# Expert rows fetched as quarters and turned by VectorE, inner rows turned among the products, attention products by form

## What is computed

```
attention:  state = gamma[h] * state + k_t v_t^T;   y_t = q_t state / sqrt(64)
experts:    e = argmax(x @ w_gate)
            out = softmax(x @ w_gate)[e] * sigmoid(x @ w_output_gate)[e] * (relu(x @ w1[e]) @ w2[e])
            w1: 8 x 512 x 1024, w2: 8 x 1024 x 512
last layer: xn = x / rms(x) * rms_g;   out = (silu(xn @ w_gate) * (xn @ w_val)) @ w_out, width 1536
```

## Time and profile before

| | us |
|---|---|
| median of 3 runs | 1125.27 |
| the runs | 1123.5 to 1125.32 |
| the profiled execution, its own time | 1125.38 |
| its span, first to last instruction | 1123.6 |
| TensorE busy in it | 1105.0 (98%) |
| attention, to the first expert product | 0 to 152 |
| expert tiles | 152 to 521 |
| last layer | 522 to the end |

### The profile page before, as it was taken

The page is one execution under the profiler, slowest core; times in us unless marked ns, Lnnn a source line. Parts: engine busy times, 40 slices in busy tenths (PEclk is TensorE's granted clock), DMA queues, the critical chain, the costliest instruction groups (busy, mean ns, idle before and its releaser), DMA issues.

```text
span 1123.6 us, 20317 instructions
## 1 busy us (share of the span) xinstructions
PE 1105.0 (98%) x6371; PEld 915.7 (81%) x6372; DVE 428.5 (38%) x804; ACT 378.3 (34%) x613; POOL 178.3 (16%) x245
## 2 busy tenths in 40 slices
PE   6999999999999999999999999999999999999998
PEld 5888887888888888787888888888888888888886
DVE  3676757433424334431433322322232232223222
ACT  2454435433434446432323212411331141132112
POOL 2444423332221200110001300200030011001000
PEclk9999999999999999999999999999999999999999
DMA  9998824524344533422201200110020001000001
GB/s 211 231 246 222 217 110 163 188 108 131 116 117 143 203 115 120 140 93 96 75 1 38 76 1 1 42 33 0 0 75 0 0 30 45 0 0 38 1 1 38
DMA packets 110996, 97.33 MB, mean 87 GB/s; under 512 B 80832, under 2 KB 86368, under 8 KB 110944
## 3 DMA queue, kind: packets, MB, share of 16 engines
q1 hardware_dynamic: 95680, 61.88, 20.4%
q0 software_dynamic: 8832, 26.81, 7.2%
q10 hardware_dynamic: 6432, 7.96, 2.0%
HBM read 76.41 MB, written 20.22 MB: 86 GB/s over the span
## 4 chain that ended last, share of the span: by engine, by line
PE 95%; DMA 3%; issue 1%; ACT 0%; POOL 0%; DVE 0%; SPq 0%; POOLq 0%; ACTq 0%
PE banks L625 15%; PE bank L701 15%; PE bank L703 15%; PE bank L702 14%; PE bank L598 14%; PE banks L701 3%; PE banks L703 3%; PE banks L702 3%; DMA x_rows<-x_out,slot_idx 3%; PE banks L494 2%; PE bank L508 2%; PE bank L538 1%; PE banks L613 1%; PE bank L589 1%; PE bank L613 1%; PE bank L670 1%
## 5 line engine op out<-in xcount | busy, mean ns | idle before, releaser
L1363 DVE TENSOR_TENSOR gated<-bank,sig 128x512 f32<-128x512 f32 x72 | 49.8, 692 | 357.6 <-ACT sig L989 357.6
L989 ACT ACTIVATE sig<-bank 128x512 f32<-128x512 f32 x72 | 43.1, 598 | 329.0 <-PE bank L703 328.9
L701 PE MATMUL bank<-xh,w1h 128*128 128x512 f32 x384 | 149.4, 389 | 0.0
L702 PE MATMUL bank<-xl,w1h 128*128 128x512 f32 x384 | 149.4, 389 | 0.0
L703 PE MATMUL bank<-xh,w1l 128*128 128x512 f32 x384 | 149.4, 389 | 0.0
L703 PEld LDWEIGHTS bank<-xh,w1l 128*128 128x128 f32 x384 | 72.1, 188 | 15.0
L702 PEld LDWEIGHTS bank<-xl,w1h 128*128 128x128 f32 x384 | 72.1, 188 | 14.9
L701 PEld LDWEIGHTS bank<-xh,w1h 128*128 128x128 f32 x384 | 72.1, 188 | 14.9
L996 ACT ACTIVATE hh<-prod 128x512 fp32r<-128x512 f32 x72 | 45.5, 632 | 110.7 <-DVE prod L1367 110.7
L1560 POOL DMA_INDIRECT out_rows<-x_out,cur_idx x10 | 10.1, 1009 | 382.3 <-ACT x_out L1003 291.4
L1372 DVE TENSOR_TENSOR hl<-prod,hh 128x512 fp32r<-128x512 f32 x72 | 49.9, 693 | 54.2 <-ACT hh L996 54.2
(11 more groups left out here) (240 smaller groups left out, 2148.0 us busy)
## 6 DMA issues: line engine op xcount, KB each, us to landing
stage<-in_moe_w SPq DMA_DIRECT2D x64, 512.0 KB, 5.4
expert_rows<-tile_o ACTq DMA_DIRECT2D x29, 256.0 KB
q_raw<-in_q SPq DMA_DIRECT2D x24, 256.0 KB, 5.4
k_raw<-in_k SPq DMA_DIRECT2D x24, 256.0 KB, 6.2
v_raw<-in_v SPq DMA_DIRECT2D x24, 256.0 KB, 4.3
stage<-in_moe_w_out SPq DMA_DIRECT2D x6, 512.0 KB, 4.1
stage<-in_moe_w_gate SPq DMA_DIRECT2D x5, 512.0 KB
stage<-in_moe_w_val SPq DMA_DIRECT2D x5, 512.0 KB, 5.8
```

Of the source, the lines that this page charges most:

```text
L701: pe.matmul(out_ap, lh, rh, start=first, stop=False)
L702: pe.matmul(out_ap, lh, rl, start=False, stop=False)
L989: nc.scalar.activation(sig[:], bank[GV[f % 2][0]][:, :], ACT.Sigmoid).then_inc(s["sig_done"], 1)
L1363: v3.tensor_tensor(gated[:], bank[GV[f % 2][0]][:, :], sig[:], ALU.mult).then_inc(s["gated_done"], 1)
```

## The change

**Rows as quarters.** The buffer `x_rows` is also read as quarter rows of 128 numbers. A fetch is now four indirect DMAs, each of 128 quarter rows (64 KB), to the four quarters of `xg`; partition p takes quarter p // 32 of rows 32 part + p % 32. Indices are computed for that (`row_idx` has four columns a tile). VectorE turns 32 x 32 blocks (four transposes of 128 x 4 x 32, `turn_rows`) into `xg_turned`, which lies in the place of `xgl`: ScalarE copies it to `xgh`, VectorE then subtracts in place. TensorE's `turn_rows` and its bank are gone. Column q * 128 + b * 32 + j of a row now lies in partition 32 q + j, block b, so the w1 pieces are loaded to match: piece b takes four stretches of 32 rows, 128 rows apart.

**Inner rows.** The first four hidden transposes stand in the middle of `up`'s second half, the other four in `down_tile` after its first four products.

**Attention.** TensorE's step is `turn_qk`, `ranks`, `outputs`, `state_sum`, `scores`, `turn_x`, `gate_logits`; VectorE copies the state before it masks the scores.

```diff
-            w1_rows = w1.rearrange("e d f -> (e d) f")
+            w1_rows = w1.rearrange("e (q b j) f -> b e q j f", q=QUARTERS, j=BLOCK)
...
             def w1_piece(at):
-                return w1_rows[ds(at * P, P), :]
+                expert, b = at
+                return w1_rows[b][ds(expert, 1)].rearrange("o q j f -> (o q) j f")
...
             def step(u):
                 turn_qk(u)
-                if u:
-                    outputs(u - 1)
                 if u > 1:
                     ranks(u - 2)
+                if u:
+                    outputs(u - 1)
+                state_sum(u)
                 scores(u)
                 if u:
                     turn_x(u - 1)
-                state_sum(u)
-                if u:
                     gate_logits(u - 1)
...
-            def turn_rows(a):
-                pe.wait_ge(s["rows_in"], 16 * (a + 1))
-                if not (isinstance(a, int) and a < 1):
-                    pe.wait_ge(s["tileT_lo"], a)
-                for i in range(KD):
-                    mm = pe.transpose(quad(XG_T)[:, i, :], xg[:, i * P:(i + 1) * P], ident)
-                mm.then_inc(s["tile_turned"], 1)
...
             def down_tile(a, at):
...
                         if wt is w2h:
                             pe.wait_ge(s["hTh" if x is hidh else "hTl"], 2 * a + g + 1)
+                        if not g and x is hidh and wt is w2l:
+                            turn_hidden(a, 1)
...
-                for g in range(2):
-                    up(a, at, g)
-                turn_hidden(a)
+                up(a, at, 0)
+                up(a, at, 1, lambda: turn_hidden(a, 0))
...
             def rows_hi(a):
-                act.wait_ge(s["tile_turned"], a + 1)
-                if not (isinstance(a, int) and a < 1):
-                    act.wait_ge(s["up_done"], 2 * a)
-                nc.scalar.activation(xgh[:], quad(XG_T), ACT.Copy).then_inc(s["tileT_hi"], 1)
+                act.wait_ge(s["tile_turned"], QUARTERS * (a + 1))
+                nc.scalar.activation(xgh[:], xg_turned[:], ACT.Copy).then_inc(s["tileT_hi"], 1)
             def turned_hi_parts(a):
                 for g in range(2):
                     if g:
-                        rows_hi(a + 1)
+                        relu(a, 1)
...
+                rows_hi(a + 1)
...
             def rows_lo(a):
                 dve.wait_ge(s["tileT_hi"], a + 1)
-                v3.tensor_tensor(xgl[:], quad(XG_T), xgh[:].bitcast(F32), ALU.subtract).then_inc(s["tileT_lo"], 1)
+                v3.tensor_tensor(xgl[:], xg_turned[:], xgh[:].bitcast(F32), ALU.subtract).then_inc(s["tileT_lo"], 1)
+            def turn_rows(a):
+                dve.wait_ge(s["rows_in"], 16 * QUARTERS * (a + 1))
+                if not (isinstance(a, int) and a < 1):
+                    dve.wait_ge(s["up_done"], 2 * a)
+                for part in range(QUARTERS):
+                    to = xg_turned[:, :, part * BLOCK:(part + 1) * BLOCK]
+                    v3.transpose(to, xg[:, part * P:(part + 1) * P].rearrange("p (b i) -> p b i", i=BLOCK))\
+                      .then_inc(s["tile_turned"], 1)
             def turned_lo_parts(a):
-                for g in range(2):
-                    if g:
-                        rows_lo(a + 1)
-                    hidden_lo_part(a, g)
+                hidden_lo_part(a, 0)
+                turn_rows(a + 1)
+                hidden_lo_part(a, 1)
+                rows_lo(a + 1)
...
             def fetch_rows(a):
...
-                nc.gpsimd.indirect_dma_start(xg[:].bitcast(U32), None, x_dram, bass.IndirectOffsetOnAxis(cur_idx[:, 0:1], 0))\
-                  .then_inc(s["rows_in"], 16)
+                for part in range(QUARTERS):
+                    nc.gpsimd.indirect_dma_start(xg[:, part * P:(part + 1) * P].bitcast(U32), None, x_quarters,
+                                                 bass.IndirectOffsetOnAxis(cur_idx[:, part:part + 1], 0))\
+                      .then_inc(s["rows_in"], 16)
```

More of the change, by code:

```diff
@@ L95, in constants @@
     a[:, A_STRICT:A_STRICT + P] = p < j
+    a[:, A_TILE:A_TILE + UNITS] = P * np.arange(UNITS)
+    a[:, A_NUM:A_NUM + TILES + 1] = np.arange(TILES + 1) - LEAD
+    a[:, A_TID:A_TID + UNITS] = P * np.arange(UNITS)[None, :] + p
+    quarter = p // BLOCK
+    rows = BLOCK * np.arange(QUARTERS)[None, None, :] + (p % BLOCK)[:, :, None]
+    for at, tiles in ((A_ROW, np.arange(TILES + 1) - LEAD), (A_LEAD, np.arange(LEAD))):
+        numbers = QUARTERS * (P * tiles[None, :, None] + rows) + quarter[:, :, None]
+        a[:, at:at + numbers[0].size] = numbers.reshape(P, -1)
+    a[:, A_QTR:A_QTR + 1] = quarter
     return c.astype(np.float32)
@@ L597, in up @@
                 for n, (x, wt, i) in enumerate(terms):
+                    if between and n == len(terms) // 2:
+                        between()
                     mm = pe.matmul(bank[(UP0, UP1)[g]][:, :], x[:, i, :], wt[:, ds(at + (i * FE + g * 512), 512)],
@@ L600, in up, with turn_hidden @@
                 mm.then_inc(s["up_done"], 1)
-            def turn_hidden(a):
-                first = isinstance(a, int) and a == 0
-                for g in range(2):
-                    if g:
-                        turn_rows(a + 1)
-                    pe.wait_ge(s["relu_done"], 2 * a + g + 1)
-                    if not first:
-                        pe.wait_ge(s["hTl"], 2 * a - 1 + g)
-                    for i in range(4):
-                        f = 4 * g + i
-                        mm = pe.transpose(quad((HT0, HT1)[g])[:, i, :], hid[:, f * P:(f + 1) * P], ident)
-                    mm.then_inc(s["h_turned"], 1)
+            def turn_hidden(a, g):
+                pe.wait_ge(s["relu_done"], 2 * a + g + 1)
+                if not (isinstance(a, int) and a == 0):
+                    pe.wait_ge(s["hTl"], 2 * a - 1 + g)
+                for i in range(4):
+                    f = 4 * g + i
+                    mm = pe.transpose(quad((HT0, HT1)[g])[:, i, :], hid[:, f * P:(f + 1) * P], ident)
+                mm.then_inc(s["h_turned"], 1)
             def down_tile(a, at):
@@ L658, in _ @@
                 pe.wait_ge(s["tileT_lo"], a + 1)
-                for g in range(2):
-                    up(a, 0, g)
-                turn_hidden(a)
+                up(a, 0, 0)
+                up(a, 0, 1, lambda: turn_hidden(a, 0))
                 down_tile(a, 0)
@@ L886, in expert_tile @@
                 store_tile(a - 1)
-                relu(a, 1)
                 turned_hi_parts(a)
@@ L899, in _ @@
             evacuate_x(UNITS - 1)
-            relu(0, 1)
             turned_hi_parts(0)
```

96 lines of the change are left out of this document (54 added, 42 removed).

## The result

The changed kernel takes 1169.1 us (median of four runs, 1169.1 to 1174.0) against 1124.6 of before: ratio 1.041, interval 1.039 to 1.043. The forecast was 1139, the range 1109 to 1157. The sign was right, the size was not: the time lies outside the range.

What follows compares the result with a forecast made beforehand. TensorE, busy 98% of the span with 95% of the chain, was taken as the bound. 1125.4 - 16.9 + 2.8 + 1.2 (tile 23's wait) + 7.3 - 2.8 = 1117.0, + 16 + 6 = 1139 us; range 1109 to 1157.

Steps and rivals of the forecast that it cites:

- The tiles, -16.9: Expert loops, 26 tiles: removing the xg transposes and a wait for hidden half 0 saves 0.65 us each, -16.9 us.
- Relu in splitting tiles, +2.8: Loop tiles that split weights: the first hidden group waits about 0.2 us for relu, +2.8 us in all.
- VectorE's turn, 0.25 each: Expert tiles: VectorE turns fetched rows in four transposes of 0.25 us, 1.0 in all, hidden in the loops.
- The lead, +7.3: Ahead of tile 2: the quarters' fetches and turns are not hidden, +7.3 us (bounds 3 and 12).
- Attention order, -2.8: Attention, 22 steps: fewer changes of form on TensorE, less later scatters, -2.8 us (-8 to +3).
- The w1 loads, +16 and +6: Four engines carry each w1 load: +16 us in attention (0 to 35), +6 at the first run change (0 to 10).
- That the loads keep their width: Rival: w1 loads are not narrowed, the other terms stand, 1117 us (1108 to 1124), faster; chance 0.35.
- The quarters are late in every tile: Rival, loop tiles: landings near 8.0 us make 13 us instead of 11.85, 1143 without w1 trouble; chance 0.07.
- The third rival: Loop tiles: the second hidden group waits 0.4 us each, 10 us go, 1127 with wide w1 loads; chance 0.06.

Runs made afterwards that it cites:

- four_one_fetch: Changed kernel with every weight piece loaded by four DMAs of 32 partitions and whole rows fetched by one indirect DMA a tile: 1116.1 us, ratio 0.993.
- four_again: Changed kernel with every weight piece loaded by four DMAs of 32 partitions, four fetches kept, run once more on chip F: 1123.3 us, ratio 0.998.
- four: Changed kernel with every weight piece loaded by four DMAs of 32 partitions, four fetches kept, on chip C: 1156.4 us, ratio 1.028.
- before_q4: Kernel before with only the w1 source changed, counted 4 x 32 rows: 1167.1 us, ratio 1.037.
- before_extra_small: Kernel before with three more indirect DMAs of 16 bytes a row behind the fetch in 14 tiles: 1124.1 us on chip E, 1124.0 on F.
- before_two_fetches: Kernel before with two indirect DMAs a tile, 64 rows each, in place of one: 1124.3 us, ratio 1.000.
- best2: Kernel before with the new attention order, hidden groups moved among the products, and ScalarE taking two pieces instead of three ahead of relu: 1118.8 us.

## Why the prediction was right or wrong

**Where the 44 us are.** Three kernels give them in steps, each step between two chips, so each is known to a few us only. With wide loads and one fetch (four_one_fetch, chip D) the tiles, the turning and the attention order are worth 1124.6 - 1116.1 = 8.5 us (9.0 against the kernel before on D itself). The four fetches cost 7.2 us where the semaphores are in time (four_again, 1123.3, chip F). The narrow loads cost the other 45.8 (1169.1, chip A); alone, in the kernel before and on one chip, they cost 42.5.

**The tiles, -16.9: right for each tile, too much in the sum.** 11.85 apart, as predicted, and tiles 9 to 17 together took 107.55 us where they took 112.53, as the two terms for them say (9 x 0.65 less 4 x 0.2 = 5.05). But between tile 2 and the last `down_tile`, the run changes apart, 4.6 us were gained and not 12.9. The six tiles from 484 us on took 77.14 instead of 77.42: they stand under a branch, and TensorE waits for its own sequencer at their start (L607, 2.6 us in 5 waits, before 0.9 in 1). I had counted these as tiles like the others. Tile 2 and tiles 4 to 8, behind the lead and the first run change, took 1.6 us more than before and not 3 to 4 less. Narrow loads are not all of it: from tile 2 to the last `down_tile` `four`, whose loads are wide, gained 4.0 us on chip F, and with one fetch 8.6 on chip D.

**Relu in splitting tiles, +2.8: right.** Two of four tiles are 12.06 to 12.08 apart, 0.22 above the others; the prediction had 0.2.

**VectorE's turn, 0.25 each: right.** The group:

```profile
L1145 DVE STREAM_TRANSPOSE xg_turned<-xg 128x128 f32<-128x128 f32 x120 | 26.6, 280 | 20.4 <-DMA xg<-x_rows,cur_idx 17.4 <-PE bank L607 2.3
```

Four take 0.89 us in the timeline, 0.22 each (the single records, 0.28 in the mean, overlap). The figure of the Trainium skill (VectorE: DVE Perf Modes, "The three transpose paths"), 0.31 for one of bf16, is what the first record of a row of four shows here for fp32; taken four times it would have been too much.

**The lead, +7.3: near in the sum, wrong in its parts.** Its first fetch is issued at 159.17 and the last quarter at 162.95, 3.8 us later as reckoned. The first expert product follows the first issue by 12.1 us and not by 9.7, since VectorE turned the rows only when its own work let it:

```profile
159.17 0.97 POOL L1454 DMA_INDIRECT xg<-x_rows,lead_idx  x1 [0.30 <-issue]
...
162.95 0.94 POOL L1454 DMA_INDIRECT xg<-x_rows,lead_idx  x1 [0.30 <-issue]
...
168.94 0.89 DVE L1145 STREAM_TRANSPOSE xg_turned<-xg 128x128 f32<-128x128 f32 x4
...
171.28 1.20 PE L607 MATMUL bank<-w1h,xgh 128*128 128x512 f32 x4 [1.28 <-DVE xgl L1137]
```

That is 5.2 us more than before and not 2.7; against that, 3.7 us and not 4.6 came after it. The runs with one fetch and with four put the price of all the quarters, tiles included, at 4.5 (1169.1 - 1164.6, two chips) and 7.2 us (1123.3 - 1116.1, two chips).

**Attention order, -2.8: right.** -3.8 by itself.

**The w1 loads, +16 and +6: the step that failed.** The mechanism was right, four engines, and its size in attention nearly: +18.9 with everything else there, against +15.9, and 18.6 to 22 from the narrow loads alone (before_q4), against +16. Mis-sized was the first run change, "+6 (0 to 10)", which took 14.3. Its own premises gave that much: three pieces, each some 7 us behind the last, are 21 us (the chain has 22.26 on `stage`), less the 5.5 of before, and relu stands on ScalarE behind all three. And "Other run changes are 36 us or more apart and hide it" was false: at 401.50 a run change stalled for another 8.7 us. With these two in their places the forecast would have been 1156; the remaining 13 us are the tiles (8.3), attention (3.0) and the last layer (2.1), less 0.9 of the lead.

**The rivals.** That the loads keep their width is refuted by 384 packets. "The quarters are late in every tile" is near what chips B, C and D show, 13.1 to 13.6 us a tile over tiles 9 to 17, but by luck: semaphores were late there, not landings. On chip A it did not happen. The third rival is refuted in the first run: the second hidden group waits nowhere for more than 0.2 us.

**What stays open.** Late semaphores were seen on chips B, C and D with four fetches, and with one on none of them (before_q4 and its like on B, three kernels on C, four_one_fetch on D), apart from single cases under 0.8 us; on A and F not even with four. Whether it is the number of the issues or what they carry stays open: before_extra_small ran on E and F and before_two_fetches on E alone, none of which has shown late semaphores with anything. What differs between the places, and whether it is the chip at all, was not tried.

## What to carry to other kernels

When an access pattern of a DMA changes, compare the outermost counts of both sides, and afterwards count the packets of its queue against before. In this case counts of 4, 8 and 16 showed 12, 8 and 0 semaphore packets fewer for each load. Reordering what each partition holds (here 4p + b instead of four blocks of 32) kept all sixteen. A term that is priced in one place, like the first run change, is worth adding up from its own premises once more, and the places that are said to hide it need the same sum. Moving a step ahead of a wait is worth only what its producer can follow; the hidden groups lost 2.7 us as they stood, and with one piece fewer ahead of relu `best2` is 2.0 us faster than the attention order alone (1118.8 and 1120.8, on two chips, their intervals overlap). A kernel that issues many indirect DMAs from GpSimd should be timed in more than one job and on more than one chip.

## What the runs showed of the hardware

Eight engines in place of sixteen for the w1 loads cost 11.5 us, four cost 42.5. On three chips kernels with four indirect DMAs a tile had semaphores between TensorE and ScalarE 0.5 to 2.4 us late, and `four` took 1156.4 us on one of them and 1123.3 on a chip where they came in time. TensorE's granted clock fell when it had stood idle: the second stall ends at 422.38 after 5.02 us without a product, and the window behind it has 0.53, close to the lower of its two levels (1.2 of 2.4 GHz). Four weight loads take 1.61 us there (423.72, above) and 0.87 at the full clock. These are that window and one with the clock back, with the columns of those above:

```profile
422.00:428.00 6.00, 5.62 (x19) 4.55 (x19) 2.81 (x6) 1.52 (x3) 0.24 (x1) 0.53 1.04 297
440.00:446.00 6.00, 6.00 (x30) 4.89 (x29) 5.29 (x10) 4.41 (x9) 2.15 (x2) 1.00 0.04 12
```

In the same 6 us TensorE ran 19 products at the lower clock, with a short wait among them, and 30 at the full one. So a long wait is paid for once more, in the products behind it.
